# Splitting w_out in block 1: high parts on ScalarE, low parts shared by GpSimd and VectorE, instead of all on VectorE

## What is computed

```python
scores = scale * np.matmul(q, k.transpose(0, 1, 3, 2))            # (2, 8, 576, 576)
kth = np.partition(scores, -32, axis=-1)[..., -32:-31]
attn = softmax(np.where(scores >= kth, scores, -1e9))
x = heads_side_by_side(np.matmul(attn, v))                        # 1152 x 512
h = x @ w_in                                                      # 1152 x 2048
g = np.maximum(h, 0.0) + alpha * np.minimum(h, 0.0)
x2 = g @ w_out                                                    # 1152 x 512
# then a gate picks 2 of 8 experts per token: relu(x2 @ w1[e]) @ w2[e], weighted and added
```

## Time and profile before

| | before |
|---|---|
| median of 3 runs | 788.92 us (788.0 to 790.17) |
| the profiled execution: its own time | 786.68 us |
| its span in the trace | 784.9 us |
| PE busy | 709.1 us, 90% of the span |
| DVE busy | 545.1 us, 69% |
| ACT busy | 408.4 us, 52% |
| POOL busy | 388.9 us, 50% |

### The profile page before, as it was taken

One profiled execution on the slowest core, in us unless ns is written; L12 is line 12 of the kernel. 1 busy time (PEld: TensorE's weight loads), 2 busy tenths in 40 slices (PEclk: granted clock), 3 DMA queues, 4 the chain that ended last, 5 costly groups with the idle time before them and its releaser, 6 DMA issues. The chain is left out here.

```text
span 784.9 us, 13266 instructions
## 1 busy us (share of the span) xinstructions
PE 709.1 (90%) x4484; PEld 537.9 (69%) x4484; DVE 545.1 (69%) x1149; ACT 408.4 (52%) x811; POOL 388.9 (50%) x288
## 2 busy tenths in 40 slices
PE   5666889899999999999999989729999999999993
PEld 2444556476675766757667566519999989999893
DVE  4999999779878798787987804663555545555520
ACT  2443554565766657666575645722535545535511
POOL 0666778476786767867678670730202202112022
PEclk9988999999999999999999999958999999999998
DMA  9593003602204032040310205364267366375322
GB/s 311 231 379 144 15 1 120 231 1 102 75 28 149 1 108 68 27 147 0 107 67 14 95 16 200 146 199 179 82 200 235 102 224 195 124 243 168 115 35 33
DMA packets 29831, 96.47 MB, mean 123 GB/s; under 512 B 5136, under 2 KB 5136, under 8 KB 28176
## 3 DMA queue, kind: packets, MB, share of 16 engines
q1 hardware_dynamic: 25408, 85.96, 30.8%
q0 software_dynamic: 4384, 9.98, 5.7%
HBM read 77.81 MB, written 37.34 MB: 147 GB/s over the span
## 5 line engine op out<-in xcount | busy, mean ns | idle before, releaser
L1232 POOL TENSOR_SCALAR scores<-scores,top 128x576 f32<-128x576 f32 x72 | 127.0, 1764 | 114.6 <-issue 47.7
L330 DVE MAX8 top<-rest 128x8 f32<-128x576 f32 x216 | 152.0, 743 | 0.0
L1323 POOL DMA_INDIRECT out_dram<-ye,xe x24 | 42.8, 1784 | 217.5 <-ACT ye L1174 212.7
L756 PE MATMUL bank<-w_in_sb,x_t 128*128 128x512 f32 x272 | 123.4, 596 | 0.0
L1234 POOL TENSOR_TENSOR expo<-scores,expo 128x576 f32<-128x576 f32 x72 | 107.7, 1496 | 6.0
L336 DVE MATCH_REPLACE8 rest<-top,rest 128x576 f32<-128x576 f32 x144 | 105.5, 738 | 0.0
L711 PE MATMUL ps_scores<-ktr,q 128*128 128x288 f32 x288 | 93.5, 452 | 11.7 <-DMA ktr<-kt_in_dram 4.7
L784 PE MATMUL bank<-w_out_high,g_parts 128*128 128x512 f32 x288 | 102.3, 416 | 1.2 <-DVE g_parts L497 0.7
L929 PE MATMUL bank<-w_hi,he_t 128*128 128x512 f32 x256 | 91.9, 400 | 0.0
L504 DVE TENSOR_TENSOR w_lo<-raw,w_hi 128x1024 fp32r<-128x1024 f32 x64 | 77.9, 1225 | 19.5 <-ACT w_hi L1121 18.6
L330 DVE MAX8 top<-scores 128x8 f32<-128x576 f32 x72 | 50.9, 747 | 50.7 <-POOL expo L1234 30.0
(11 more groups left out here) (164 smaller groups left out, 1305.4 us busy)
## 6 DMA issues: line engine op xcount, KB each, us to landing
raw<-w_dram SPq DMA_DIRECT2D x64, 512.0 KB, 9.3
x_sorted_dram<-x_sorted_dram SPq DMA_DIRECT2D x7, 2570.0 KB, 10.6
q<-qz_dram SPq DMA_DIRECT2D x18, 256.0 KB, 2.7
xe<-x_sorted_dram SPq DMA_DIRECT2D x8, 514.0 KB, 4.8
w_in_sb<-w_in_dram SPq DMA_DIRECT2D x4, 1024.0 KB, 8.5
w_out_raw<-w_out_dram SPq DMA_DIRECT2D x4, 1024.0 KB, 8.4
out_dram<-x_now SPq DMA_DIRECT2D x1, 3584.0 KB, 28.3
x_sorted_dram<-x_now SPq DMA_DIRECT2D x1, 2570.0 KB, 19.1
```

Of the source, the lines that this page charges most:

```text
L330: nc.vector.max(dst, src).then_inc(chain if r < ROUNDS - 1 else dve_top, 1)
L756: mm = pe.matmul(dst, x_t[:, k, :], w_in_sb[:, k, c * 512:(c + 1) * 512], start=(k == 0), stop=(k == MK - 1))
L1232: nc.gpsimd.tensor_scalar(mask, mask, top[:, n % 4, TOPK - 1:TOPK], None, ALU.is_ge).then_inc(pool_mask, 1)
```

## The change

`split_w_out` is gone. `high_w_out(c)` on ACT makes the high part of quarter c in two pieces of 1024 columns, at h = c of block 1, behind that head's exponential. `low_w_out(piece)` makes the low part of one piece: POOL makes the even pieces (0, 2, 4, 6) at h = 0 to 3, each behind that head's probabilities, and DVE the odd ones: piece 1 behind pair 1, pieces 3 and 5 behind pair 2, piece 7 behind pair 3. Both wait for the piece's high part (`act_w_high`). PE's second layer of block 0 waits for both low parts.

```diff
+SPLIT_AT = {0: 0, 1: 1, 2: 2, 3: 3}
+SPLIT_PAIRS = {1: (0,), 2: (1, 2), 3: (3,)}
...
-            def split_w_out(c):
-
-                dve.wait_ge(w_out_in, 64)
-                at = slice(4 * c * MODEL, 4 * (c + 1) * MODEL)
-                nc.vector.tensor_copy(w_out_high[:, at], w_out_raw[:, at]).then_inc(dve_w_high, 1)
-                dve.wait_ge(dve_w_high, c + 1)
+            def low_w_out(piece):
+
+                dve.wait_ge(act_w_high, piece + 1)
+                at = slice(piece * PIECE, (piece + 1) * PIECE)
                 nc.vector.tensor_tensor(w_out_low[:, at], w_out_raw[:, at], w_out_high[:, at].bitcast(F32),
                                         ALU.subtract).then_inc(dve_w_low, 1)
...
                     topk_pair(HEADS * blk + 2 * pair, 2 * pair)
-                    if split:
-                        split_w_out(pair)
                     if pair == (0 if split else 1) and not first:
                         row_sums(blk - 1, 1)
+                    if split and pair in SPLIT_PAIRS:
+                        for c in SPLIT_PAIRS[pair]:
+                            low_w_out(2 * c + 1)
...
                 if isinstance(j, int) and j == 0:
                     pe.wait_ge(dve_w_low, c + 1)
+                    pe.wait_ge(pool_w_low, c + 1)
...
+            def high_w_out(c):
+
+                if c == 0:
+                    act.wait_ge(w_out_in, 64)
+                for piece in (2 * c, 2 * c + 1):
+                    at = slice(piece * PIECE, (piece + 1) * PIECE)
+                    nc.scalar.copy(w_out_high[:, at], w_out_raw[:, at]).then_inc(act_w_high, 1)
...
                     if not (last and h + 2 >= HEADS):
                         exp_tile(tile + 2, h + 2, PAIRS * blk + (h + 2) // 2 + 1)
+                    if split and h in SPLIT_AT:
+                        high_w_out(SPLIT_AT[h])
...
+            def low_w_out(piece):
+
+                pool.wait_ge(act_w_high, piece + 1)
+                at = slice(piece * PIECE, (piece + 1) * PIECE)
+                nc.gpsimd.tensor_tensor(w_out_low[:, at], w_out_raw[:, at], w_out_high[:, at].bitcast(F32),
+                                        ALU.subtract).then_inc(pool_w_low, 1)
...
                     if mlp and h in GATE_G_AT:
                         prelu(blk - 1, GATE_G_AT[h])
+                    if split and h in SPLIT_AT:
+                        low_w_out(2 * SPLIT_AT[h])
```

More of the change, by code:

```diff
@@ L220, in moe_program @@
         dve_g_low = sem("dve_g_low")
-        dve_w_high = sem("dve_w_high")
+        act_w_high = sem("act_w_high")
         dve_w_low = sem("dve_w_low")
+        pool_w_low = sem("pool_w_low")
         act_h1 = sem("act_h1")
@@ L1067, in copy_gates, with one_block @@
                 nc.scalar.copy(dst, src[:, 0:2 * EXPERTS]).then_inc(act_gate, 1)
-            def one_block(blk, mlp=True, gate=True, last=False):
+            def high_w_out(c):
[4 more added lines that the diff above has]
+                    nc.scalar.copy(w_out_high[:, at], w_out_raw[:, at]).then_inc(act_w_high, 1)
+            def one_block(blk, mlp=True, gate=True, last=False, split=False):
                 for h in range(HEADS):
@@ L1098, in _ @@
             one_block(0, mlp=False, gate=False)
-            one_block(1, gate=False)
+            one_block(1, gate=False, split=True)
             one_block(2)
@@ L1253, in low_g, with one_block @@
                                         g_parts[:, c % 2, 0, :].bitcast(F32), ALU.subtract).then_inc(pool_g_low, 1)
-            def one_block(blk, mlp=True, first=False):
+            def low_w_out(piece):
[3 more added lines that the diff above has]
+                                        ALU.subtract).then_inc(pool_w_low, 1)
+            def one_block(blk, mlp=True, first=False, split=False):
                 for h in range(HEADS):
@@ L1274, in _ @@
                                     ALU.subtract).then_inc(alpha_ready, 1)
-            one_block(1, first=True)
+            one_block(1, first=True, split=True)
             with pool.Fori(2, BLOCKS) as blk:
```

## The result

The changed kernel takes 809.17 us (median of 4 runs, 807.94 to 810.39) against 788.69 for the kernel before. The ratio is 1.0257, with a 95% interval of 1.0233 to 1.0281: 20 us slower. The forecast was 807, range 801 to 812. The profiled execution spans 806.5 us, 21.6 more than before.

A forecast was written before the change was run, and what follows sets the result against it. It took DVE to bound block 1 and PE the later blocks; a new loop through POOL, PE and ACT would delay tile 16 by 18.3 us, so 786.7 + 18.3 = 805.0, plus 2.2 for the median: 807, range 801 to 812.

The forecast's parts named there:

- The loop: Block 1, heads 0 to 3: POOL's subtraction waits for ACT's cast, which waits via PE for POOL's last tile; 803 to 810, chance 0.62.
- The turns: Four passes POOL, PE, ACT, POOL in block 1, each x(h) + 6.75 us, together 51.0 us (63.6 to 114.6).
- x(h): Block 1, head h: time from the end of tile 8+h's probabilities to ACT's exponential's end; 4.7, 5.7, 6.8, 6.8 us.
- POOL's subtraction: POOL's low part of 1024 columns in block 1, four times: 2.4 us each, together 9.6 us.
- P(8): End of POOL's probabilities product for tile 8, block 1's start: 63.6 instead of 65.84, a gain of 2.2 us.
- DVE against POOL: Block 1: cost to POOL of DVE subtractions beside its masks; taken as 0, at most 3.6 us; exclusion rival 811 us, chance 0.12.
- the mask's row: Earlier trace, POOL's mask at 103.79 beside a DVE subtraction: read as DVE losing only 0.4 us and POOL 0.
- From tile 12 to tile 16: End of block 1: POOL runs at block 2's spacing, from 114.6 to 140.5 us.
- The sum: Whole kernel: profiled 786.7 + 18.3 = 805.0, and 2.2 more for the median of runs: 807.2, rounded to 807.
- The mark: Start of PE's transposes of tile 16: from 122.33 to 140.6, 18.3 us later.
- Part given back: Rival: warm PE starts in block 1 or block 2's 3.78 us queries' wait recover some loss; 797 to 803, chance 0.15.
- The way that DVE's gain could go through: Rival: casts ready before POOL asks in block 1, DVE's 10.4 us saved, 778.5; chance 0.04 faster, 0.03 within 0.3%.

The follow-up runs named there:

- cast_first: Changed kernel with ACT's two casts of each quarter moved to the start of the head, ahead of its wait for PE: 783.88 us, ratio 0.9924 to the kernel before.
- pool_later: Changed kernel with POOL's four subtractions one head later, ACT's casts left in place: 784.78 us, ratio 0.9938 to the kernel before.
- pool_memset: Changed kernel with POOL's four subtractions replaced by fills with zeros behind the same waits: 799.34 us, ratio 1.0143 to the kernel before.
- two_turns: Changed kernel with POOL's subtractions at heads 0, 1, 3 and 4 instead of 0 to 3: 796.76 us, ratio 1.0107 to the kernel before.
- dve_memset: Changed kernel with DVE's four subtractions replaced by fills with zeros, POOL subtracting as before: 807.48 us, ratio 1.0226 to the kernel before.
- no_pool: Changed kernel with DVE making all low parts in whole quarters and POOL none, ACT's casts unchanged: 781.67 us, ratio 0.9902 to the kernel before.
- no_pool_spread: Same as no_pool, but DVE's subtraction of quarter 2 stands behind pair 3 instead of pair 2: 782.65 us, ratio 0.994 to the kernel before.
- spread: Changed kernel with ACT's casts at head starts, POOL's pieces at heads 1, 2, 5, 6, DVE's behind pairs 1, 2, 3, 3: 780.41 us, ratio 0.9889.

## Why the prediction was right, and where its sizes were off

- **The loop.** Right, in place and in size. The turns took 12.0, 12.4, 14.3 and 14.6 us (P(9) 76.26, P(10) 88.69, P(11) 102.95, P(12) 117.57) where I had 11.4, 12.5, 13.5 and 13.6. cast_first and pool_later open it from either side and end below the kernel before with the same work; pool_memset keeps the wait, cuts POOL's added work from 9.4 to 3.8 us and stays 11 us above it; two_turns frees one passage of the four, 3.2 us instead of 14.3, and the loss falls from 20.3 to 8.4 us.
- **x(h).** From P(8+h) to the end of the exponential it took 4.5, 5.4, 6.8 and 7.1 us against 4.7, 5.7, 6.8 and 6.8. Taking the starts of PE as after a wait was right: its clock in block 1 fell from 0.92 of full in the earlier trace rows to 0.79, and the four transposes take 1.11 or 1.12 us at tiles 9 to 12, as they had at tile 10 before. In the 3 us or so from each of them the granted clock was 0.50 to 0.53, the 1.2 GHz level, after PE had stood idle for 3.3 to 7.8 us; in the 3 us from tile 16's it was 1.00, and they took 0.63 us. Cast and handoff took 1.0 instead of 1.15.
- **POOL's subtraction.** 2.36 us against the 2.4 read off the slope between 512 and 576 columns.
- **P(8).** The gain on the mask and product was there: 1.72 and 1.41, so 3.2 us as taken. The mask started 0.6 us later (61.00 against 60.44); POOL's product ahead of it had done so already (55.59 against 55.02), before anything that was changed.
- **DVE against POOL.** The mis-sized term. I took 0, by the mask's row; it measured 0.97, 0.98 and 0.97 on three masks and 0.42 on a product, 3.3 us in all, close to the 3.6 that I gave as the other end. dve_memset shows the cause. I had read a mask that was already running when DVE's subtraction came: there DVE lost 0.4. But the next row of the same timeline had the price, which I passed over: the product of tile 14, behind that mask, took 2.33 us instead of 1.41, and DVE's subtraction had ended 1.08 us into it, at 107.65.

```profile
106.57 2.33 POOL L1234 TENSOR_TENSOR expo<-scores,expo 128x576 f32<-128x576 f32 x1
```

The Trainium skill, SBUF — State Buffer, section "Who interferes with whom", calls the port pair that DVE and GpSimd share an exclusive lock, which the first to issue holds for its whole instruction. By that rule the sum had been 21.9, against 20.8 measured. The traces agree with it where DVE's subtraction comes first (2.69 instead of 1.72), and not where POOL's mask runs first (0.4 lost by DVE, not the rest of the mask).

In the changed kernel the order is the other way about. DVE's subtraction comes up while POOL's own subtraction runs, waits for its end (2.52 us for piece 5 instead of 1.20), and gets in ahead of the mask, which then waits for it.
- **From tile 12 to tile 16.** 25.5 us against 25.9: block 2's spacing carried over.
- **The sum.** The mark came at 143.12, 2.5 us later than 140.6: +2.35 from the turns (53.35 against 51.0: +3.3 for the masks and the product, -1.0 for the smaller terms), +0.6 from the late start, -0.4 from the last four heads. So the 807 came out near the 809.17 in part because small terms, each taken a little high, made up for a third of the collisions.
- **Part given back.** It was not. The queries' wait of tile 24 is 4.57 us against 3.78; it moved with `copy_x2`, 19.0 us behind it as before (19.2).
- **Not foreseen.** DVE's wait of 9.9 us ahead of piece 5 for ACT's cast. It makes no pair later in the changed kernel, because DVE waits another 3.33 us for P(11) behind it.
- **The way that DVE's gain could go through.** cast_first shows it partly: the loop opened, but only 5.6 us (789.49 less 783.88) came of the 10.4. What stops the rest was not predicted. Up to P(12) it gained only 1.7 us (93.22 against 94.92), with the wait of 3.49 us and the 2.0 us that the mask of tile 12 was held ahead of it; from P(12) to P(16) it took 25.4 us instead of 27.3.

In the first four heads DVE is still the bound of no_pool, no_pool_spread and spread: it has no gap there, and POOL stands idle for it ahead of the mask of tile 12 (4.83, 4.83 and 3.27 us). What stays open is the limit behind tile 12. That POOL is on the path from there, as no_pool_spread took it, is not shown. No version without any collision between DVE and POOL was tried.

## What to carry to other kernels

Moving work to idle engines is priced by where the waits land in each program, not by sums of busy time: a share that waits for a product of the same step it stands behind closes a loop, and every turn then takes the whole round trip (12 to 14.6 us here, where a head had taken 7.3 on average, for 2.4 us of work). Put the producer's share ahead of its engine's own wait, or the consumer's share one step later. When DVE and POOL share the work, look in the trace for what each kind of DVE instruction does to the POOL instruction behind it (here a subtraction and a cast held it, a fill didn't), and count that as time on POOL whenever POOL is on the path.

## What the runs showed of the hardware

- A DVE subtraction of two SBUF operands and a POOL mask that comes up behind it hardly overlap: the mask took 2.69 us behind one of 1.2 us, 5.98 behind two of 2048 columns, and 1.72 beside a DVE fill. Behind a DVE cast of 1.20 us it took 2.70 in the kernel before. Where DVE's subtraction had come up during POOL's, it got in before POOL's next instruction in each case seen. But a mask that was running first cost DVE's subtraction only 0.4 us in the kernel before, of 1.56 us side by side, and the mask lost nothing, so the exclusion is not whole in that order.
- A POOL subtraction of 1024 columns takes 2.36 us, a POOL fill of the same 0.95, and ACT's cast 1.04.
